# Attention stage of a fused kernel issued in another order, with two sets of folded tokens and the first layer norm's scaling on VectorE

## The reference, cut to what matters

```python
kv = einsum('bhsd,bhse->bhde', k, v)                 # linear attention: a 64x64 matrix per head
out = einsum('bhsd,bhde->bhse', q, kv)
x = out / sqrt(mean(out*out, -1) + 1e-6) * g_norm    # per token and head
u = x + real(fft(fft(x, axis=tokens), axis=features))
un = (u - mean(u)) / sqrt(var(u) + 1e-6)
x2 = u + relu(un @ w_ch1) @ w_ch2                    # w_ch1 512x2048, w_ch2 2048x512
u2 = x2 + V.T @ (U.T @ x2)  (rank 32, over tokens)
result = u2 + relu(u2 @ moe2_w_ch1) @ moe2_w_ch2
```

## Time and profile before

| | us |
|---|---|
| median of 3 runs (1755.22 to 1761.6) | 1757.88 |
| the profiled execution, its own time | 1755.45 |
| its span | 1753.6 |
| TensorE busy, share of the span | 1699.4, 97% |
| VectorE busy | 1377.0, 79% |
| ScalarE busy | 805.9, 46% |
| GpSimd busy | 237.1, 14% |
| span up to the first product of the layers | 235.15 |

### The profile page before, as it was taken

How to read it: one execution, slowest core, us unless ns; L and a number is a source line. 1 busy time by engine, 2 the same in 40 slices (tenths; PEclk the granted TensorE clock), 3 DMA queues, 4 the chain that set the end, 5 groups by cost and what they waited for, 6 DMA issues and landing times.

```text
span 1753.6 us, 27424 instructions
## 1 busy us (share of the span) xinstructions
PE 1699.4 (97%) x10712; PEld 1645.8 (94%) x10712; DVE 1377.0 (79%) x1734; ACT 805.9 (46%) x1169; POOL 237.1 (14%) x171
## 2 busy tenths in 40 slices
PE   6999999899999999999999999999999999999999
PEld 5877789889999999999999999999999999999999
DVE  4999988988888887987976867956857758658567
ACT  1444555545445445445445445435434444443343
POOL 0474340020020020020110110100100100100200
PEclk8999999999999999999999999999999999999999
DMA  7677569998898898898886777966867767767663
GB/s 239 237 246 232 203 230 354 373 356 299 315 336 304 325 318 302 323 315 315 321 283 248 282 228 265 348 229 241 277 222 254 264 229 255 265 221 254 229 248 124
DMA packets 124321, 478.15 MB, mean 273 GB/s; under 512 B 13089, under 2 KB 47201, under 8 KB 83618
## 3 DMA queue, kind: packets, MB, share of 16 engines
q1 hardware_dynamic: 121762, 475.22, 77.3%
q10 hardware_dynamic: 2432, 1.18, 0.3%
HBM read 396.14 MB, written 78.64 MB: 271 GB/s over the span
## 4 chain that ended last, share of the span: by engine, by line
PE 75%; DVE 17%; issue 4%; ACT 1%; DMA 1%; SPq 1%; POOL 1%; DVEq 0%; ACTq 0%
PE pair L958 11%; PE pair L960 11%; PE pair L959 11%; PE pair L989 6%; PE pair L991 6%; PE pair L990 6%; PE pair L978 5%; PE pair L981 5%; PE pair L980 5%; DVE t_lo L1610 3%; DVE t_raw L1629 2%; PE pair L736 2%; DVE w_sb L1538 1%; PE tr_ps L846 1%; PE pair L757 1%
## 5 line engine op out<-in xcount | busy, mean ns | idle before, releaser
L958 PE MATMUL pair<-t_hi,w_sb 128*128 128x384 f32 x1344 | 461.4, 343 | 10.8 <-DVE h_sb L1647 7.2
L959 PE MATMUL pair<-t_lo,w_sb 128*128 128x384 f32 x1344 | 455.9, 339 | 0.0
L960 PE MATMUL pair<-t_hi,w_sb 128*128 128x384 f32 x1344 | 455.6, 339 | 0.0
L1291 ACT ACTIVATE t_hi<-t_raw 128x768 fp32r<-128x768 f32 x240 | 203.1, 847 | 280.0 <-DVE t_raw L1629 279.9
L1610 DVE TENSOR_TENSOR t_lo<-t_raw,t_hi 128x768 fp32r<-128x768 f32 x300 | 302.9, 1015 | 17.7 <-ACT t_hi L1279 16.4
L1856 POOL TENSOR_TENSOR t_raw<-a_sb 128x768 f32<-128x768 f32 x60 | 138.6, 2313 | 1267.0 <-PE pair L981 553.0
L978 PE MATMUL pair<-w_sb,t_hi 128*128 128x256 f32 x1008 | 285.4, 283 | 8.5 <-DVE t_lo L1610 7.9
L980 PE MATMUL pair<-w_sb,t_hi 128*128 128x256 f32 x1008 | 282.6, 280 | 0.0
L981 PE MATMUL pair<-w_sb,t_lo 128*128 128x256 f32 x1008 | 282.5, 280 | 0.0
L958 PEld LDWEIGHTS pair<-t_hi,w_sb 128*128 128x128 f32 x1344 | 252.8, 188 | 19.4 <-issue 14.9
L959 PEld LDWEIGHTS pair<-t_lo,w_sb 128*128 128x128 f32 x1344 | 253.0, 188 | 2.6
(11 more groups left out here) (187 smaller groups left out, 2218.7 us busy)
## 6 DMA issues: line engine op xcount, KB each, us to landing
w_sb<-wc SPq DMA_DIRECT2D x263, 1024.0 KB, 5.4
wc<-w_sb SPq DMA_DIRECT2D x25, 1024.0 KB, 6.3
w_raw<-wr1a SPq DMA_DIRECT2D x24, 512.0 KB, 6.6
w_raw<-wr1b SPq DMA_DIRECT2D x24, 512.0 KB, 4.0
w_raw<-wr2a SPq DMA_DIRECT2D x10, 1024.0 KB, 7.7
wc<-pb_v SPq DMA_DIRECT2D x16, 640.0 KB, 7.0
u_dram<-x_sb SPq DMA_DIRECT2D x24, 384.0 KB, 5.5
res_sb<-u_dram SPq DMA_DIRECT2D x36, 256.0 KB, 7.4
```

Source lines behind the costliest of these rows:

```text
L958: nc.tensor.matmul(ps, w_hi, hi[:, x, :], start=(fresh and x == 0), stop=False, skip_group_check=True)
L959: nc.tensor.matmul(ps, w_hi, lo[:, x, :], start=False, stop=False, skip_group_check=True)
L960: last = nc.tensor.matmul(ps, w_lo, hi[:, x, :], start=False, stop=(x == 1), skip_group_check=True)
L1291: nc.scalar.activation(t_hi[r][:, :, :], t_raw[r][:, :, :], ACT.Copy).then_inc(hi_ready, 1)
```

## The change

All engines of the attention stage get another order; nothing is added to or removed from the arithmetic of a batch. `more` is true in steps 1 to 6.

TensorE:

```diff
             def phase1_step(b, first, more):
-                attention(b, (0, 1), False, late=not first)
+                attention(b, (1, 2), False, late=not first)
+                if more and not first:
+                    kv_products(b + 1)
                 seq_transform(b - 1, first)
-                attention(b, (2,), False)
+                if first:
+                    kv_products(b + 1)
                 if more:
-                    kv_products(b + 1)
-                feature_transform(b - 1, first)
+                    attention(b + 1, (0,), False)
+                feature_transform(b - 1, first, more)
-            kv_products(0)
-            attention(0, (0, 1), True)
+            first_kv_products()
+            attention(0, (0, 1, 2), True)
             kv_products(1)
-            attention(0, (2,), True)
+            attention(1, (0,), False)
```

VectorE (`weigh` is the multiplication by `g_norm`, cut out of `normalise`; there are two sets of `ce_sb` and `so_sb` now, for even and odd batches, so `fold_features(b)` waits for the products of batch b-2):

```diff
             def phase1_step(b, first, more):
-                sums(b, 0)
                 sums(b, 1)
-                normalise(b, 0)
+                sums(b, 2)
                 normalise(b, 1)
+                normalise(b, 2)
+                for g in range(NT):
+                    weigh(b, g)
+                if not first:
+                    fix_row(b - 2)
                 fold(b, 0, False)
-                if not more:
+                fold(b, 1, False)
+                if more:
+                    fold_tokens(b, 2, False)
+                    unfold(b - 1, 0, first)
+                    sums(b + 1, 0)
+                    unfold(b - 1, 1, first)
+                    normalise(b + 1, 0)
+                    unfold(b - 1, 2, first)
+                    fold_features(b, 2, False)
+                    for n in SUMMED.get(b, ()):
+                        split_unit_lo(UNITS[n])
+                else:
+                    fold(b, 2, False)
+                    for t in range(NT):
+                        unfold(b - 1, t, first)
                     ln_scale()
-                sums(b, 2)
-                normalise(b, 2)
-                if more:
-                    fold_tokens(b, 1, False)
-                    unfold(b - 1, 0, first)
-                    fold_features(b, 1, False)
-                    unfold(b - 1, 1, first)
-                    fold(b, 2, False)
-                else:
-                    fold(b, 1, False)
-                    fold(b, 2, False)
-                    unfold(b - 1, 0, first)
-                    unfold(b - 1, 1, first)
-                unfold(b - 1, 2, first)
-                fix_row(b - 1)
-                for n in SUMMED.get(b, ()):
-                    split_unit_lo(UNITS[n])
+                    for q in range(NCH):
+                        ln_apply(q)
+                    fix_row(b - 1)
```

`ln_apply` is a TENSOR_SCALAR of VectorE now, and ScalarE's six are gone. ScalarE's step:

```diff
+                square(b, 1, False)
+                square(b, 2, False)
+                root(b, 1)
+                root(b, 2)
+                if more and not first:
+                    copy_kv(b + 1)
+                for s in range(4):
+                    copy_seq(b - 1, (s,))
+                    if not more:
+                        ln_square(s)
+                copy_row(b)
+                copy_g(b - 1)
+                if first:
+                    copy_kv(b + 1)
+                if more:
+                    square(b + 1, 0, False)
+                copy_cos(b - 1, 0, first)
+                copy_cos(b - 1, 1, first)
+                if more:
+                    root(b + 1, 0)
+                copy_cos(b - 1, 2, first)
+                if not more:
+                    ln_total(4)
...
```

SyncE: the first k and v come as whole tiles of tokens (rows of 2 KB) instead of pairs of heads (pieces of 512 B), the third pair of k and v stands ahead of the first units, and four constants move to ScalarE's queue:

```diff
-            for n in range(NP):
-                cols = slice(128 * n, 128 * (n + 1))
-                sp.dma_start(k_sb[0][:, 0:4, cols], k_main[0][:, :, cols]).then_inc(kv0_loaded[n], 16)
-                sp.dma_start(k_sb[0][0:64, 4, cols], k_rest[0][:, cols]).then_inc(kv0_loaded[n], 16)
+            for t in range(4):
+                sp.dma_start(k_sb[0][:, t, :], k_main[0][:, t, :]).then_inc(kv0_loaded[t], 16)
+            sp.dma_start(k_sb[0][0:64, 4, :], k_rest[0]).then_inc(kv0_loaded[4], 16)
...
             load_kv(1)
             load_q(1)
-            sp.dma_start(cseq_sb[:, :, :], c_seq).then_inc(const_loaded, 16)
-            sp.dma_start(sseq_sb[:, :, :], s_seq).then_inc(const_loaded, 16)
-            sp.dma_start(cft_sb[:, :, :], c_feat).then_inc(const_loaded, 16)
-            sp.dma_start(sft_sb[:, :, :], s_feat).then_inc(const_loaded, 16)
-            sp.dma_start(ident[:, :], eye).then_inc(const_loaded, 16)
+            load_kv(2)
             load_unit(UNITS[0])
             load_unit(UNITS[1])
+            sp.dma_start(ident[:, :], eye).then_inc(eye_loaded, 16)
```

More of the change, by code:

```diff
@@ L340, in sem @@
             return ctx.enter_context(nc.semaphore(name))
-        const_loaded = sem("const_loaded")
+        const_loaded, feat_loaded, eye_loaded = sem("const_loaded"), sem("feat_loaded"), sem("eye_loaded")
         gn_loaded = sem("gn_loaded")
-        kv0_loaded, q0_loaded = [[sem(f"{what}0_loaded{n}") for n in range(m)] for what, m in (("kv", NP), ("q", NT))]
+        kv0_loaded, q0_loaded = [[sem(f"{what}0_loaded{n}") for n in range(m)] for what, m in (("kv", 5), ("q", NT))]
         kv_loaded, q_loaded = [[sem(f"{what}_loaded_{r}") for r in range(2)] for what in ("kv", "q")]
@@ L724, in _, with first_kv_products @@
         def _(pe):
+            def first_kv_products():
+                for t in range(5):
+                    pe.wait_ge(kv0_loaded[t], 32)
+                    rows = 128 if t < 4 else 64
+                    for h in range(NP):
+                        cols = slice(128 * h, 128 * (h + 1))
+                        last = nc.tensor.matmul(kv_ps[:, cols], k_sb[0][0:rows, t, cols], v_sb[0][0:rows, t, cols],
+                                                start=(t == 0 and h == 0), stop=(t == 4), skip_group_check=True)
+                last.then_inc(kv_summed, 1)
             def kv_products(b):
                 r = b % 2
-                if b:
-                    pe.wait_ge(kv_loaded[r], 64 * ((b + 1) // 2))
-                    pe.wait_ge(kv_copied, 2 * b)
+                pe.wait_ge(kv_loaded[r], 64 * ((b + 1) // 2))
+                pe.wait_ge(kv_copied, 2 * b)
                 for h in range(NP):
-                    if b == 0:
-                        pe.wait_ge(kv0_loaded[h], 64)
                     cols = slice(128 * h, 128 * (h + 1))
@@ L799, in last_seq_part @@
                     rows = PT + 1 if t == 0 else PT
-                    last = nc.tensor.matmul(ps[:, 0:KC], ce_sb[0:rows, t, 128 * dt:128 * (dt + 1)],
+                    last = nc.tensor.matmul(ps[:, 0:KC], ce_sb[(B - 1) % 2][0:rows, t, 128 * dt:128 * (dt + 1)],
                                             cseq_sb[0:rows, t, :], start=(t == 0), stop=(t == NT - 1))
@@ L1223, in phase1_step @@
                         ln_total(q)
-            for n in range(NP):
-                cols = slice(128 * n, 128 * (n + 1))
-                act.dma_start(v_sb[0][:, 0:4, cols], v_main[0][:, :, cols]).then_inc(kv0_loaded[n], 16)
-                act.dma_start(v_sb[0][0:64, 4, cols], v_rest[0][:, cols]).then_inc(kv0_loaded[n], 16)
+            for t in range(4):
+                act.dma_start(v_sb[0][:, t, :], v_main[0][:, t, :]).then_inc(kv0_loaded[t], 16)
+            act.dma_start(v_sb[0][0:64, 4, :], v_rest[0]).then_inc(kv0_loaded[4], 16)
             act.wait_ge(warm_zeroed, 1)
@@ L1345, in turn_gathered @@
                 nc.scalar.activation(gt_sb[0:64, P, :], gt_ps[0:64, :], ACT.Copy).then_inc(gt_hi_ready, 1)
-            for q in range(NCH):
-                ln_apply(q)
-                if q:
-                    take_in(q - 1, first_tr_ps[(q - 1) % 2])
-            take_in(NCH - 1, first_tr_ps[1])
-            copy_seq(B - 1, (0, 1, 2, 3))
+            copy_seq(B - 1, LAST_SEQ)
+            take_in(0, first_tr_ps[0])
+            take_in(1, first_tr_ps[1])
+            copy_g(B - 1)
+            for q in range(2, NCH):
+                take_in(q, first_tr_ps[q % 2])
+            copy_cos(B - 1, 0, False)
             hi_up(0, 0)
-            copy_g(B - 1)
+            copy_cos(B - 1, 1, False)
             hi_up(0, 1)
             split_slot_hi(1)
-            for t in range(NT):
-                copy_cos(B - 1, t, False)
+            copy_cos(B - 1, 2, False)
             for g in range(NG):
@@ L1497, in ln_scale, with ln_apply @@
                 nc.vector.tensor_tensor(ln_shift[:, :], ln_mean[:, :], ln_ri[:, :], ALU.mult).then_inc(ln_shifted, 1)
+            def ln_apply(q):
+                dve.wait_ge(ln_shifted, 1)
+                u = in_buffer(q)
+                nc.vector.tensor_scalar(u[:, :], u[:, :], ln_ri[:, q:q + 1], ln_shift[:, q:q + 1],
+                                        ALU.mult, ALU.add).then_inc(in_ready, 1)
             def split_unit_lo(unit):
@@ L1721, in add_transform @@
                 last.then_inc(u_added, 1)
-            for t in range(NT):
-                unfold(B - 1, t, False)
-                if t == 0:
```

(15 more changed lines are left out.)

128 lines of the change are left out of this document (49 added, 79 removed).

## The result

The changed kernel takes 1777.63 us (median of 4 runs, 1774.84 to 1786.14), against 1758.02 (4 runs) for the kernel before: a ratio of 1.0122, with a 95% interval of 1.0097 to 1.0147, in which the quotient of the two medians, 1.0112, lies too. It is 19.6 us slower. The profiled execution took 1776.28 us, its span is 1774.4 us, the mean granted clock 0.985.

A forecast was written before the change was run, and what follows sets the result against it. It took TensorE as the bound behind 235.15 us and TensorE and VectorE as both nearly full in the attention stage. Gains of 0.9 + 2.2 - 1.6 = 1.5 us off 1757.9 gave 1756.4, range 1746 to 1764.

The forecast's parts named there:

- prologue: Stretch up to the token products of step 2: gain of 0.9 us, ends gain 7 and loss 1.5 (late landing).
- passage: From token products of step 7 to the second product step: 42.4 us against 40.8, loss 1.6, ends +1.5 and -5.
- P: Start of attention(b, (1, 2)) in step b, the mark from which times in a step are counted.
- The recut of the first loads: Loads of batch 0 in long rows at 328 GB/s, not 512 B pieces at 290: saves 0.9 us in the prologue.
- Steps 2 to 6: Five steps of the attention stage: 126.0 us against 128.2, gain 2.2; ends gain 6.4 and loss 5.7.
- The ring through SyncE's queue: Loop of fix_row, store, loads, products; fix_row to landing 15.3 us with a weights unit, 13.7 without.
- step 3: Attention step: waits 2.0 us for k and v of batch 4, plus 1.5 for the slow clock: 27.6 us.
- Step 5: Attention step without a weights unit ahead; k and v land at 28.7 against 28.3 needed: 24.9 us.
- the clock's: 1.5 us added in step 3, from a granted clock of 0.54 for 3.5 us behind an earlier 2.2 us wait.
- Rival 2: Loads bound each second step: steps -5.7, prologue -1.5, passage -1.6, in all 8.8 us slower, 1766.7; chance 0.16.
- Rival 3: Contention with GpSimd stays, VectorE at 25.1 us a step: steps 129.0, in all 1.5 slower, 1759.4; chance 0.09.
- Rival 1: The order works: k, v in time in steps 3 to 6, prologue less cold; gain 8.8 us, 1749.1; chance 0.33.

The follow-up runs named there:

- kernel 1: The changed kernel with the load of cseq_sb (97 partitions) cut into rows 0 to 95 and row 96: 1767.7 us, ratio 1.0064.
- kernel 3: The changed kernel with the cseq_sb load cut in two and loads of k and v ahead of the stores of u: 1752.91 us, ratio 0.9981.
- kernel 5: The kernel before with the load of cseq_sb cut into 96 and 1 partitions, still on SyncE: 1755.18 us, ratio 0.9997.
- kernel 4: The kernel before with its four constants issued by ScalarE in place of SyncE: 1772.8 us, ratio 1.0095.
- kernel 7: kernel 3 with the first two loads of the layers' weights ahead of store_u(5) in SyncE's queue: 1751.13 us, ratio 0.9966.
- kernel 8: kernel 7 with fold(0, 1) ahead of sums(1, 0) and normalise(1, 0) in VectorE's prologue: 1746.71 us, ratio 0.9949.
- kernel 2: The changed kernel with each load of k and v one place earlier in SyncE's queue, ahead of the store of u: 1763.25 us, ratio 1.0038.
- kernel 6: The changed kernel with fix_row(b - 2) first in VectorE's step instead of behind the weighing: 1757.39 us, ratio 1.0012.

## Why the prediction was wrong

The forecast was 1756.4 us, the range ended at 1764, and the time is 1777.6. It added up +0.9 (prologue), +2.2 (steps) and -1.6 (passage); measured are -10.3, -10.2 and -1.6, with 1.3 back in the loop. Two terms failed, by 11.2 and by 12.4 us: the first for a mechanism that it didn't have, the second by its sizes.

- **The prologue: a mechanism that was missing.** It forecast a gain of 0.9 with a late end of 1.5; the loss was 10.3. The step was "0.67 MB of constants ... now run on ScalarE's queue beside these loads", priced as bandwidth alone, 2.0 and 1.6 us. What was missed is that an issue is also an instruction in ScalarE's own program, and can itself be held, and that what stands behind such a load lands late. Kernels 1, 3 and 5 show the first: split, the block goes and the P of step 2 comes 7.4 and 8.6 us earlier; taken out in the kernel before from SyncE, it changes nothing. Kernel 4 shows both, the late landing above all. The bandwidth, which was priced, was priced well: where the block is gone (kernels 1, 3, 7 and 8), the products of batch 1 wait for k and v until 24.7 to 26.3, for a forecast of 24.0 between 22.8 and 26.4. The hold stood in the trace of before, in the 12.38 us row shown under kernel 5. It was in sight and not carried along with the instruction that it belonged to. With the measured 10.3 in that term the forecast would have been 1756.4 + 11.2 = 1767.6, beyond the upper end of the range and still 10 short.
- **The recut of the first loads**, priced at 0.9 us: attention of batch 0 starts at 13.3 to 14.2 us in the seven kernels with whole tiles, and at 15.0, 15.6 and 17.4 in the three with pieces of 512 B. The direction holds; no run changed the cut alone.
- **Why that load.** The runs show that an issue behind a load of 97 partitions waits 11.6 to 15.4 us, and 0.32 us behind the same load cut into 96 and 1. The Trainium skill (DMA: Bandwidth & Descriptors, Why a DMA increments its semaphore by 16 and not by 1) says that a transfer is spread over the largest number of engines, up to 16, that divides the slowest dimension of both its sides: 97 is a prime, so one engine carries all of it, and 96 takes 16. The traces agree with that rule, as the split shows: 1.9% of 16 engines in ScalarE's queue with the one load, 24.6% with the two. That the next issue is then held, as in kernel 5's rows, that section's rule doesn't say by itself, and why it is held no run here tells. Other sizes of the load than 97 and 96 + 1 were not run.
- **Steps 2 to 6: right mechanism, wrong sizes.** The ring through SyncE's queue, a wait in step 3 and a step with room behind it: as worked out. Step 5 was to be 24.9 us, within the 24 to 25 that the forecast named as its sign, and took 34.2. Step 3 waited 3.9 us and not 2.0: 1.1 because fix_row to landing took 16.4 us and not 15.3, 0.6 because a step without a wait is 24.1 and not 24.6 us long, so that k and v are needed earlier. (15.3 was short by the forecast's own rows: 14.85 us for 3.8 MB and 0.26 MB more at 328 GB/s make 15.6.) Step 5 waited 3.6 and not 0.4, in the same way, with 16.1 for 13.7. The term that was mis-sized most is the clock's: 1.5 us were added behind step 3's wait, by a stretch at 0.54 of 3.5 us, where its products lost 4.35 (10.17 for 5.82), and at most the few tenths that its 24.9 us hold beyond the wait in step 5, where 4.4 and 2.1 were lost: 1.5 to 2 us for 10.8. Thus step 3 took 32.2 (27.6 forecast) and step 5 34.2 (24.9), in sum 138.4 for 126.0.
- **A hit that was luck.** fix_row was to be done at P + 15.0 and was, at 15.1. But the weighing began at P + 9.2 (10.6 in the forecast) and took 5.27 us (3.65): two errors of about 1.5 us that cancel.
- **Rival 2, "the loads become the bound"**, was the right one for the steps, and its price too small: -5.7 there, -10.2 measured. It was to decide "from about 17 us on"; 16.1 to 16.4 were enough, since the 40 products behind a wait lost more by the low clock than the wait was long.
- **Steps without waits**: 24.6 was forecast for one with a unit. They take 24.1, in all kernels that have no wait for k and v: TensorE's work alone.
- **Rival 3, contention**, was half right. The copies of two elements are back at 158 ns, but the weighing went from 792 to 940 ns. VectorE still ends in time, so the steps don't get longer by it directly, as kernel 3 shows. But in steps 2 and 4 of the kernel after, the weighing stands ahead of fix_row, and its 5.27 us in place of 3.69 put the ring back by 1.6 us each time. That the waits of 3.9 and 3.6 us would be so much shorter without it is an estimate; no run took it away.
- **The passage**: forecast P + 44.2 and a loss of 1.6; measured P + 44.3 and 1.6, with the weights' sum at P + 28.0 ahead of it. Kernel 7 takes that wait away and gets 1.2 of it back. That the total is met so closely is in part luck: with the same code the passage took 47.8 us in kernel 1's trace.
- **What the changed order is worth.** In kernel 3, without both faults, the second product step comes 4.6 us earlier than before (234.09 against 238.69). That is the order's own worth: 7.9 us from the steps, less 1.6 in the prologue and 1.8 in the passage. Its median is 4.6 us below the kernel before. Rival 1's 8.8 for the order as drawn was reached by none but kernel 8, with two more edits.

Open stays what the cost behind a wait depends on. Its length alone doesn't give it. Waits for k and v and the 40 products behind them, in us: 1.28 and 6.08 (kernel 8), 1.29 and 6.08 (kernel 3), 1.64 and 7.98 (kernel 7), 1.67 and 10.40, 4.55 and 7.63, 3.56 and 9.18 (kernel 1), 3.58 and 10.19, 3.90 and 10.17 (the kernel after).

## What to carry to other kernels

Before a DMA issue is moved to another engine, read how long the issue itself took where it stood, ask what compute stands behind it in its new program, and how long the queue is that it joins. A load of 97 partitions is cut into 96 and 1; by the rule of the Trainium skill named above the same would hold for any count that has no large divisor up to 16, which no run here tried. And where a store and a load share a queue, what the store waits for is also what the load waits for: when its producer moves, count the time from there to the landing, and price the products behind a wait up to their length at the lower clock (here up to 10.4 us for 5.8), not the wait alone.

## What was not expected of the hardware

- One blocked issue can hold a compute engine for 15.4 us (ScalarE), and the time differs from trace to trace: 15.39, 12.93 and 12.95 us for the same load in the new order (the kernel after, kernels 2 and 6), 11.61 in the old one (kernel 4). With no such load in any queue, an issue of SyncE's behind a long queue was held for 11.88 us (kernel 1).
- How much VectorE is stretched beside GpSimd's additions depends on the instruction. In step 3 of the kernel after, the weighing, which reads and writes SBUF, took 940 ns for 680 undisturbed, while in the same step the normalising multiplication out of PSUM took 682 ns on the average.
- Waits of 3.6 and 3.9 us in the kernel after were followed by 14 and 9 us at a granted clock near 0.50. A wait of 1.3 us in kernel 8's prologue was not: its 40 products took 6.08 us. But one of 1.67 us in kernel 1's was: they took 10.40.
